# TensorE's middle loop of the first layer: written out three times, or a loop of the chip

## The reference

```
for t in range(S):                                  # B, H, S, D = 4, 8, 768, 48
    state = alpha[t][..., None] * state + outer(k[t], v[t])
    y[t]  = q[t] @ state
x = y as (3072 tokens, 384)
x = (sigmoid(x @ w_gate) * (x @ w_val)) @ w_out     # d_ff 1536
x = max(x @ w1, x @ w2, x @ w3) @ w_out2            # d_ff 768
```

## Time and profile before

| | us |
|---|---|
| median of 3 runs | 884.87 (884.81 to 885.73) |
| the profiled execution | 884.87 |
| its span | 883.1 |
| TensorE busy in the span | 854.5 |
| VectorE, ScalarE, GpSimd busy | 413.1, 262.6, 120.8 |

### The profile page before, as it was taken

One profiled execution on the slowest core, in us unless ns is written; L12 is line 12 of the kernel. 1 busy time (PEld: TensorE's weight loads), 2 busy tenths in 40 slices (PEclk: granted clock), 3 DMA queues, 4 the chain that ended last, 5 costly groups with the idle time before them and its releaser, 6 DMA issues.

```text
span 883.1 us, 13792 instructions
## 1 busy us (share of the span) xinstructions
PE 854.5 (97%) x5405; PEld 797.2 (90%) x5405; DVE 413.1 (47%) x730; ACT 262.6 (30%) x502; POOL 120.8 (14%) x95
## 2 busy tenths in 40 slices
PE   4599999999999999999999999999999999999997
PEld 3499999999999999999999999988888888888886
DVE  7888566366456456555555532232323232232321
ACT  3534333232332332233232233421312222121311
POOL 3355412011011011111111103600000000000000
PEclk9889999999999999999999999999999999999999
DMA  7481021021021021021021021300000000000000
GB/s 300 140 332 46 7 90 46 7 91 46 3 94 45 1 97 45 1 97 45 1 97 45 1 79 38 107 1 1 16 21 1 36 0 36 0 36 0 23 12 36
DMA packets 15599, 46.83 MB, mean 53 GB/s; under 512 B 2112, under 2 KB 6080, under 8 KB 15552
## 3 DMA queue, kind: packets, MB, share of 16 engines
q1 hardware_dynamic: 15552, 46.15, 14.8%
HBM read 40.24 MB, written 4.72 MB: 51 GB/s over the span
## 4 chain that ended last, share of the span: by engine, by line
PE 95%; DVE 3%; ACT 1%; DMA 0%; issue 0%; POOL 0%; SPq 0%; DVEq 0%; ACTq 0%; POOLq 0%
PE ps_out L824 17%; PE ps_val L799 17%; PE ps_gate L799 17%; PE ps_gate L805 8%; PE ps_val L805 8%; PE ps_out L896 6%; PE ps_sc L799 6%; PE ps_y L788 3%; PE ps_sc L757 3%; PE ps_sc L805 3%; PE ps_y L784 2%; PE ps_sc_odd L896 2%; PE ps_y L741 1%; PE ps_sc L767 1%; DVE rdec L566 1%; DMA cst<-consts 0%
## 5 line engine op out<-in xcount | busy, mean ns | idle before, releaser
L799 PE MATMUL ps_gate<-x_hi,w_hi 128*128 128x384 f32 (+1 forms) x396 | 139.6, 353 | 1.8 <-ACT x_hi L387 1.8
L799 PE MATMUL ps_val<-x_hi,w_hi 128*128 128x384 f32 (+1 forms) x396 | 140.5, 355 | 0.3 <-DVE h_sb L629 0.3
L799 PE MATMUL ps_gate<-x_hi,w_lo 128*128 128x384 f32 (+1 forms) x396 | 139.1, 351 | 0.0
L799 PE MATMUL ps_val<-x_hi,w_lo 128*128 128x384 f32 (+1 forms) x396 | 138.6, 350 | 0.0
L805 PE MATMUL ps_gate<-x_lo,w_hi 128*128 128x384 f32 (+1 forms) x396 | 118.1, 352 | 0.0
L805 PE MATMUL ps_val<-x_lo,w_hi 128*128 128x384 f32 (+1 forms) x396 | 117.0, 349 | 0.0
L629 DVE TENSOR_TENSOR h_sb<-act_sb,ps_val 128x384 f32<-128x384 f32 x96 | 52.6, 548 | 135.2 <-PE ps_val L805 135.1
L387 ACT ACTIVATE h_hi<-h_sb 128x384 fp32r<-128x384 f32 x96 | 50.4, 525 | 160.0 <-DVE h_sb L629 159.9
L428 ACT ACTIVATE act_sb<-ps_gate 128x384 f32<-128x384 f32 x96 | 47.2, 492 | 149.6 <-PE ps_gate L805 149.3
L714 DVE TENSOR_TENSOR probs<-probs,ps_val 128x512 f32<-128x512 f32 x36 | 24.7, 686 | 137.8 <-PE ps_val L805 137.8
L566 DVE RECIPROCAL rdec<-decay 112x128 f32<-112x128 f32 x96 | 85.7, 923 | 0.5
(11 more groups left out here) (98 smaller groups left out, 1246.9 us busy)
## 6 DMA issues: line engine op xcount, KB each, us to landing
inbuf<-att_in SPq DMA_DIRECT2D x23, 704.0 KB, 5.6
mid<-w SPq DMA_DIRECT2D x12, 576.0 KB, 9.2
inbuf<-att_in SPq DMA_DIRECT2D x23, 256.0 KB, 2.8
mid<-alpha_flat SPq DMA_DIRECT2D x8, 576.0 KB, 7.2
inbuf<-w SPq DMA_DIRECT2D x6, 768.0 KB, 4.2
out<-inbuf SPq DMA_DIRECT2D x5, 768.0 KB, 3.5
x_raw<-y_last SPq DMA_DIRECT2D x48, 24.0 KB, 1.9
out<-inbuf SPq DMA_DIRECT2D x4, 192.0 KB, 2.1
```

The source lines that it names most:

```text
L799: mm(bank, w_at(half, f, c + k * P, total=total), x_hi[:, k, 0:w], start=(k == 0 and half == 0), stop=False)
```

## The change

TensorE's loop over tiles 1 to 6 becomes a `Fori` of three turns. Nothing else is edited, and the matmuls, their operands and their order are the same. With it, the counter `i` of `layer1`, `scores`, `transposes`, `attend`, `outer` and `out1` is a register for these tiles, as it was already on the other four engines.

```diff
             layer1(0, 0, True, False)
-            for i in range((TILES - 2) // 2):
+            with pe.Fori(0, (TILES - 2) // 2) as i:
                 for Ts in (1, 2):
                     layer1(Ts, i, True, True)
             layer1(TILES - 1, 0, False, True)
```

## The result

| | before | after |
|---|---|---|
| median | 884.84 us (884.75 to 885.73) | 893.61 us (892.06 to 894.14, four runs) |
| the profiled execution | 884.87 | 890.85 |
| its span | 883.1 | 889.1 |

The ratio is 1.0094, with a 95% interval from 1.0077 to 1.0111: the loop makes the kernel 8.8 us slower. The forecast of 885.0 was wrong, and so was its range. The profiled execution of the changed kernel was itself 2.8 us shorter than the median of the others; experiment 9 shows why.

A forecast was written before the change was run, and what follows sets the result against it. TensorE, busy for 854.5 of 883.1 us, was taken to bound the kernel. Nothing removed, 0.1 us for registers and 0 for branches on 884.87 us gave 885.0 us, range 884.0 to 892.0.

The forecast's parts named there:

- What bounds the kernel: Tiles 1 to 6: TensorE is busy throughout, so whatever holds it up lengthens the run.
- Removed: Two of three body copies and their code transfers on q8: nothing on the path goes away, 0 us.
- Added, 1: Waits in the three turns compare with register values computed on TensorE's sequencer: 0.1 us, from 0 to 4.5 us.
- rival C: Attention parts: register waits hold up the 18 chunks, the 0.25 us pause at the scores doubles, 889.4 us; chance 0.12.
- Added, 2: Two taken branches back, after tiles 2 and 4: target not resident and fetched each time, but covered, 0 us for both.
- Price of a fetch: Code fetch at each branch back: 2.1 us, from 0 to 4.2 us, taken from small data transfers.
- Cover of a fetch: At each branch back, the sequencer is 4.3 to 8.3 us ahead of the array, hiding the fetch.
- The sum: Whole kernel: 884.87 + 0.1 for registers + 0 for branches = 885.0 us.
- Rival B: Turn starts after tiles 2 and 4: the branch back is exposed, 889.1, 893.3 or, with lower clock, 896.9 us; chance 0.27.
- A: Whole kernel: no change, register waits and branches without a price, 885.0 us, own range 884.2 to 886.6; chance 0.57.
- What would show it: Turns of tiles 1-2, 3-4, 5-6 take 136.1 us each, TensorE busy throughout; wrong if one takes 137 us or more.

The follow-up runs named there:

- experiment 9: The changed kernel run once more with no further edit, to trace another execution: 895.76 us beside 884.88 for the kernel before.
- experiment 1: Changed kernel with the body written out three times, its counter computed from a register, no branch taken: 884.93 us, ratio 0.9998 to the kernel before.
- experiment 7: Layer 2's loop of the kernel before at 970 instructions, 884.91 us; changed kernel with matmuls left out, 1817 and 1241 instructions a turn, 816.41 and 785.16 us.
- experiment 3: Changed kernel with SyncE's attention loads moved away from the branch: 887.05 us, ratio 1.0025; the same move in the kernel before: 884.92 us.
- experiment 8: Changed kernel with one taken branch, the turn ending inside a tile behind `outer` of f = 3: 893.25 us, ratio 1.0087 to the kernel before.
- experiment 2: Changed kernel with tiles 5 and 6 written out, one branch back in place of two: 889.14 us, ratio 1.0049 to the kernel before.
- experiment 4: Changed kernel with the language's hint on the loop's back edge: 889.59 us, ratio 1.0050 to the kernel before.
- experiment 5: Changed kernel with both the back-edge hint and SyncE's attention loads moved away from the branch: 889.03 us, ratio 1.0040 to the kernel before.

## Why the prediction was wrong

**What bounds the kernel** was right: TensorE has no slack there, and each of its stops is in the time.

**Removed: 0 us.** Right, and moot. In the second turn of after q8 has 10 transfers where the earlier trace rows has 8.

**Added, 1: 0.1 us for the registers.** Right (experiment 1), and rival C falls with it. The reading of layer 2's turns against its tile 0 was sound.

**Added, 2: is the target at hand?** "I take it that it is not" was right (5.5 us against 0.22), and so was reading that from the count of instructions. A loop of 1241 would have stayed. By the 2048 instructions that the prediction cites, one of 1817 would have stayed too; it did not (experiment 7), so "just too large" is right only in its direction.

**"Price of a fetch", 2.1 us with 4.2 as the upper end: the step that failed first.** Measured: 3.5 and 3.8 us with nothing else on the queues, 5.5 and 5.8 with the loads. The packet itself was sized well (0.93 us of one engine; 0.9 to 1.3 in experiment 3), but the landing time of a small data transfer is not the price of a missed branch: with nothing else on the queues 0.9 us pass before the packet starts and 1.5 behind its end, and the prediction has no term for either (experiment 3). The upper end was missed too, because the loads that start just before the branch were not put beside it. The earlier trace rows give the queue's mean share, 0.14, over a turn; in the 1.5 us from 247.0 it is 0.5, and 0.9 in the stop.

**"Cover of a fetch", 4.3 to 8.3 us: the step that failed second.** Measured: 3.0 us, below its lower end. The lower end asked only what the sequencer waits for, and took it to run freely up to the branch once `h_lo` was finished at 246.07. It does not: it holds 17 matmuls, 34 instructions with their weight loads, and met the branch at 247.5. The upper end came from the moment of a code transfer, which is a block brought ahead and tells nothing of where the sequencer stands. What would have told it was in the trace of before: the branch of layer 2's loop stands there with its start, 674.2, and the turn ends at 677.55, with the same 17 matmuls between. The row also has the 215 ns of a branch that hits.

The Trainium skill (TensorE: Matmul & The Clock Gate, engine queue depths) gives 64 entries, from which the prediction worked out an estimate of 5.5 us. The traces show 17 matmuls, 34 instructions with their weight loads, still to come at branches of three different loops (lines 927 of before, 879 of after and 884 of experiment 8); by what they show, 3.0 us is the figure.

**The sum.** With the measured terms, 5.8 - 3.0 + 0.3 = 3.1 and 5.5 - 3.0 + 0.3 = 2.8 us make 5.9 and 890.8, the first trace. Where the clock falls behind the stops, the three turns are 8.7 longer (experiment 9): 884.9 + 8.7 = 893.6, the median. That the four executions of the median went that way is inferred from this agreement; none of them has a trace. Rival B named the place, the sign of it ("idle time of PE before the first gate product of tiles 3 and 5, named as issue") and the clock, and gave 896.9 with the clock in both. Its chance of 0.27 was too low: the two numbers that should decide between A and B, price and cover, were both taken from rows of something else, and both erred to the side of A. The range left out the clock, which fell behind such stops in five of six traces.

**What would show it.** "I am wrong if a turn takes 137 us or more" was the right test: 139.15 and 138.93.

## What to carry to other kernels

In these runs a loop on TensorE cost nothing that can be measured as long as its turn stayed in the engine's instruction memory (970 and 1241 instructions did, 1817 did not), whatever its waits compare with. Beyond that, each taken branch cost 3.5 to 5.8 us less the time of 17 matmuls (fewer where TensorE waits for others), and often a lower clock behind it: put the branch behind long matmuls and away from loads, hint it with an outcome that is also right at the exit, or write the loop out. Before a branch is priced, look up the sequencer's own branch rows; they give its duration and, against the next matmul, the cover.

## What the runs showed of the hardware

- A taken branch of TensorE lasts 207 to 238 ns when its target is in memory, 338 to 388 ns when a hint has fetched it, 3.5 to 3.8 us when the code packet meets no loads (experiments 3, 7 with 1817 instructions, and 8), 5.3 to 5.8 us behind loads of 256 to 704 KB that are issued just before the branch. One that falls through lasts 76 to 88 ns.
- A hint that is wrong at the exit moves the price there: 2.35 and 2.62 us, behind the fifth matmul of the code that follows the loop, with weight loads on the queues in both.
- Stops of 2.4 to 3.4 us were followed by a granted clock of 0.50 to 0.59 in five of the six traces with such a stop (experiments 2, 4, 5, 8 and 9), and not in the first trace of after. The stops of 0.9 us and less in the two traces that have them (experiments 3 and 7) were not.
- A stop can be named after a semaphore (`x_hi`) and still be a late branch; the branch's end, 0.2 to 0.3 us before the matmul, shows it.
